# Expert products of a routed attention block: the first product with weights stationary and 512 tokens moving, in tiles of 512 or 384 tokens

## The reference

```python
# attention: 4 batches x 8 heads, 576 positions, 64 wide
scores = q @ k.T / 8;  keep scores >= rowmax - tau;  softmax over the kept;  x = probs @ v
x = x.transpose(0, 2, 1, 3).reshape(2304, 512)
# routed experts: 8 experts, one chosen for each token
logits = x @ w_gate + modality_bias[modality_id];  e_idx = argmax(logits)
for e in range(8):
    mask = e_idx == e
    h = np.maximum(x[mask] @ w1[e], 0.0)          # 512 -> 1024
    out[mask] = gate_w[mask, None] * (h @ w2[e])  # 1024 -> 512
# last stage, all tokens
h = out @ w_in;  g = h * tanh(softplus(h));  return g @ w_out   # 512 -> 2048 -> 512
```

## Time and profile before

| | us |
|---|---|
| median of 3 runs | 943.39 |
| lowest, highest | 942.22, 945.95 |
| the profiled execution, its own time | 944.29 |
| its span | 942.5 |
| PE busy in the span | 911.8 (97%) |
| DVE, ACT, POOL busy | 659.5, 540.9, 474.5 |

### The profile page before, as it was taken

One profiled execution on the slowest core, in us unless ns is written; L12 is line 12 of the kernel. 1 busy time (PEld: TensorE's weight loads), 2 busy tenths in 40 slices (PEclk: granted clock), 3 DMA queues, 4 the chain that ended last, 5 costly groups with the idle time before them and its releaser, 6 DMA issues.

```text
span 942.5 us, 19883 instructions
## 1 busy us (share of the span) xinstructions
PE 911.8 (97%) x7120; PEld 764.8 (81%) x7121; DVE 659.5 (70%) x1179; ACT 540.9 (57%) x1147; POOL 474.5 (50%) x560
## 2 busy tenths in 40 slices
PE   6999999999899999999999989999999999999996
PEld 4777777777678788888877978898889898889985
DVE  7989999998855411111153898888888788788793
ACT  5898898999862322222255465545555455455552
POOL 5232244656512763000000586777776777777884
PEclk9999999999999999999999999999999999999999
DMA  4131337342216563111234100001001000000000
GB/s 131 53 103 53 103 128 260 104 131 69 74 36 200 180 230 81 47 37 46 70 132 177 43 1 3 33 34 34 23 12 35 35 1 1 34 1 1 34 1 34
DMA packets 21940, 66.00 MB, mean 70 GB/s; under 512 B 3553, under 2 KB 3553, under 8 KB 21601
## 3 DMA queue, kind: packets, MB, share of 16 engines
q1 hardware_dynamic: 14512, 39.90, 12.6%
q0 software_dynamic: 4896, 20.00, 6.3%
q10 hardware_dynamic: 2448, 5.01, 1.8%
HBM read 46.63 MB, written 18.27 MB: 69 GB/s over the span
## 4 chain that ended last, share of the span: by engine, by line
PE 61%; DVE 5%; issue 3%; ACT 1%; DMA 1%; ACTq 1%; POOL 0%; DVEq 0%; POOLq 0%; SPq 0%
PE psum L1424 6%; PE psum L1426 6%; PE psum L1425 6%; PE psum L1416 6%; PE psum L1414 6%; PE psum L1415 6%; PE psum L1087 3%; PE psum L1089 3%; PE psum L1088 3%; PE psum L1114 3%; PE psum L1116 3%; PE psum L1115 3%; DVE rr L1536 2%; PE psum L1098 2%; PE psum L1073 1%
## 5 line engine op out<-in xcount | busy, mean ns | idle before, releaser
L1536 DVE RECIPROCAL rr<-rr 128x384 f32<-128x384 f32 x96 | 244.1, 2543 | 10.0 <-ACT rr L1484 10.0
L1362 POOL TENSOR_TENSOR uu<-uu,ex 128x384 f32<-128x384 f32 x96 | 97.5, 1015 | 100.5 <-ACT uu L1478 100.5
L1414 PE MATMUL psum<-x2T_hi,w_in_hi 128*128 128x384 f32 x384 | 131.0, 341 | 4.3 <-DVE gg L1542 2.7
L1416 PE MATMUL psum<-x2T_hi,w_in_lo 128*128 128x384 f32 x384 | 129.7, 338 | 0.0
L1415 PE MATMUL psum<-x2T_lo,w_in_hi 128*128 128x384 f32 x384 | 129.1, 336 | 0.0
L716 DVE TENSOR_SCALAR_CACHE_REDUCE ssb<-psum,tauk 128x576 f32<-128x576 f32 x144 | 112.6, 815 | 21.5 <-PE psum L418 16.5
L564 ACT ACTIVATE prob<-ssb,smin 128x576 f32<-128x576 f32 x144 | 113.0, 787 | 23.6 <-DVE ssb L716 22.8
L1168 DVE TENSOR_TENSOR hT_lo<-psum,hT_hi 128x512 fp32r<-128x512 f32 x38 | 26.3, 691 | 140.5 <-ACT hT_hi L1145 135.5
L1484 ACT ACTIVATE rr<-uu 128x384 f32<-128x384 f32 x96 | 50.5, 526 | 118.8 <-POOL uu L1362 118.8
L1424 PE MATMUL psum<-w_hi,g_hi 128*128 128x512 f32 x288 | 114.5, 398 | 0.1
L1425 PE MATMUL psum<-w_lo,g_hi 128*128 128x512 f32 x288 | 114.0, 396 | 0.0
(11 more groups left out here) (201 smaller groups left out, 2124.0 us busy)
## 6 DMA issues: line engine op xcount, KB each, us to landing
qk<-in_qk_dram SPq DMA_DIRECT2D x15, 640.0 KB, 3.9
vsb<-in_v_dram SPq DMA_DIRECT2D x16, 512.0 KB, 3.7
xrow<-xs ACTq DMA_DIRECT2D x17, 288.0 KB, 2.9
ys<-ysb SPq DMA_DIRECT2D x19, 257.0 KB, 3.2
stage<-in_w_in_dram POOLq DMA_DIRECT2D x16, 256.0 KB, 4.3
wa<-in_wa_dram SPq DMA_DIRECT2D x8, 512.0 KB, 7.8
wb<-in_wb_dram SPq DMA_DIRECT2D x8, 512.0 KB, 11.2
xs<-zrow SPq DMA_DIRECT2D x11, 288.0 KB, 3.1
```

The costliest lines, as they stand in the source:

```text
L1414: pe.matmul(bank_of(n), w_in_hi[:, k, cols], xT_hi[w][:, k], start=(k == 0), stop=False)
L1416: last = pe.matmul(bank_of(n), w_in_lo[:, k, cols], xT_hi[w][:, k], start=False, stop=(k == KT - 1))
L1536: dve.reciprocal(rr[:, n % 4], rr[:, n % 4]).then_inc(r_done, 1)
```

## The change

The first product of the experts is turned around: a block of 128 x 128 of w1 is stationary and up to 512 tokens move, so h comes out with features in rows, as the second product needs it. `turn_h` and its transposes go; the relu and the high half become one ACT operation, `max(h, 0) - high` one DVE operation. Tiles have 512 tokens (`LEAD_W` = 4 blocks of 128) for the lead and 384 (`OTHER_W` = 3) for the others. One tile (instead of three) is worked on early. The rows of a tile are loaded as four blocks, each with its own register load and transfer, always four. There is one buffer for the rows (`xrow`, four blocks), one for the results (`ysb`, four blocks) and a small one for the gates, which are copied over when the previous results have been stored. The halves of the turned x are made by four copies and four subtractions, one for each 128 features, and those of the next tile are made at the end of a tile, after its last first product.

Two loops: one over the lead's tiles, one over the other experts. The w2 pass for the lead goes; POOL now makes the low half of w2. w_in is loaded in four transfers of 1 MB into the place of its low half and split there. The last stage's first chunks of `ys` (`yrow`) now lie where the expert rows lay, so POOL waits for the last turned rows and gates before it loads them, and PE waits for the last expert result before the first product of the last stage, not the eighth. Four blocks of `xs` are cleared instead of three, and the table computation on DVE has some ten small operations more.

```diff
-EARLY = 3
+LEAD_W, OTHER_W = 4, 3
+EARLY = 1
...
-        for i in range(EARLY):
+        for i in range(LEAD_W):
             row = sp.value_load(tab["early"][0:1, i:i + 1], min_val=i * P, max_val=(E - 1) * CAP + i * P)
-            early["load_row"](sp, i, row)
+            early["load_block"](sp, i, row)
...
+    def load_block(eng, j, row):
+        eng.dma_start(xrow[:, j], io["xs"][bass.ds(row, P), :]).then_inc(x_in, 16)
     def load_x(eng, i):
-        load_row(eng, i, eng.value_load(tab["rows"][0:1, 0, bass.ds(i, 1)], min_val=0, max_val=E * CAP - P))
+        eng.wait_ge(x_turned, KT * i)
+        eng.wait_ge(gate_done, i)
+        for j in range(LEAD_W):
+            load_block(eng, j, eng.value_load(tab["rows"][0:1, j, bass.ds(i, 1)], min_val=0, max_val=E * CAP - P))
...
-                pe.matmul(h_bank[:, half, :], xT_hi[:, k], w1h[:, k, c], start=(k == 0), stop=False)
-                pe.matmul(h_bank[:, half, :], xT_hi[:, k], w1l[:, k, c], start=False, stop=False)
-                last = pe.matmul(h_bank[:, half, :], xT_lo[:, k], w1h[:, k, c],
-                                 start=False, stop=(k == KT - 1))
+                pe.matmul(out, w1h[:, k, cols], xT_hi[:, k, q], start=(k == 0), stop=False)
+                pe.matmul(out, w1h[:, k, cols], xT_lo[:, k, q], start=False, stop=False)
+                last = pe.matmul(out, w1l[:, k, cols], xT_hi[:, k, q], start=False, stop=(k == KT - 1))
...
-        def turn_h(i, half):
-            pe.wait_ge(relu_done, 2 * i + 1 + half)
-            for k in range(half_f):
-                f = half * half_f + k
-                last = pe.transpose(ht_bank[:, half, k * P:(k + 1) * P], hid[:, f * P:(f + 1) * P], ident[:])
-            last.then_inc(h_turned, 1)
...
+        def rest_of_tile(i, f0, wide, w1_split, w2_split):
+            for f in range(f0, FT1):
+                if f == FT1 - 1:
+                    turn_x(i + 1, 0)
+                    turn_x(i + 1, 1)
+                up(i, f, wide, w1_split)
+                if f >= 2:
+                    down(i, f - 2, wide, w2_split)
+            turn_x(i + 1, 2)
+            down(i, FT1 - 2, wide, w2_split)
+            turn_x(i + 1, 3)
+            down(i, FT1 - 1, wide, w2_split)
...
+        def tile(i, wide):                    # ACT
+            load_x(act, i + 1)
+            h_hi(i, 0, wide)
+            evacuate_y(i)
+            for f in range(1, FT1):
+                h_hi(i, f, wide)
+            for k in range(KT):
+                x_hi(i + 1, k)
+            move_gates(i)
+            gate_of(i + 1)
...
+        pool.wait_ge(y_stored, 16 * first_rows + 16)
+        pool.wait_ge(x_turned, KT * (tiles + 1))
+        pool.wait_ge(gate_done, tiles + 1)
         for c in range(2):
+            if c == 1:
+                pool.wait_ge(y_stored, 16 * tiles + 16)
+                pool.wait_ge(x_out, KT * (tiles + 1))
...
-            if n == AHEAD - 1:
+            if n == 0:
                 pe.wait_ge(y_out, tiles)
```

More of the change, by code:

```diff
@@ L547, in tensor @@
         rows_out(NS - 2)
[L548 to L555, removed]
+        up(0, 1, LEAD_W, 0, {1: lambda: rows_out(NS - 1)})
+        up(0, 2, LEAD_W, 0)
+        down(0, 0, LEAD_W, 0)
+        ranks(B - 1)
+        up(0, 3, LEAD_W, 0)
+        down(0, 1, LEAD_W, 0)
+        pe.wait_ge(ranks_read, B)
+        rest_of_tile(0, 4, LEAD_W, 0, 0)
     def scalar(act):
@@ L652, in scalar @@
         normalise(NS - 1)
-        h_hi(0, 0)
-        relu(0, 1)
-        x_hi(1)
-        gate_of(1)
[L657 to L668, removed]
+        h_hi(0, 1, LEAD_W)
+        h_hi(0, 2, LEAD_W)
+        gate_exps(B - 1)
+        for f in range(3, FT1):
+            h_hi(0, f, LEAD_W)
+        for k in range(KT):
+            x_hi(1, k)
+        move_gates(0)
+        gate_of(1)
     def vector(dve):
@@ new lines, in gpsimd @@
+        tiles, ranks = counts(pool)
+        first_rows = pool.value_load(tab["counts"][0:1, 2:3], min_val=1, max_val=TILES_MAX)
+        with pool.Fori(1, ranks) as r:
+            for k in range(WP):
+                cols = slice(k * PIECE, (k + 1) * PIECE)
+                pool.wait_ge(w2_hi_done, WP * r + (k + 1))
+                pool.tensor_tensor(w2_lo[:, cols], wb[:, cols], w2_hi[:, cols].bitcast(F32),
+                                   ALU.subtract).then_inc(w2_ready, 1)
+        pool.wait_ge(y_stored, 16 * first_rows + 16)
@@ L1076, in up_half, with turn_x @@
-        def up_half(i, half, split, between={}):
-            c = slice(half * 512, (half + 1) * 512)
-            if half == 0:
-                pe.wait_ge(x_out, i + 1)
-            for k in range(KT):
-                if half == 0:
+        def turn_x(i, k):
+            if k == 0:
+                pe.wait_ge(x_in, 16 * LEAD_W * i + 16 * LEAD_W)
+            if k == KT - 1 or (k == 2 and not first_tile(i)):
+                pe.wait_ge(x_out, KT * i + (1 if first_tile(i) else k - 1))
+            cols = slice(2 * k * HW + E, 2 * k * HW + E + P)
+            for j in range(LEAD_W):
+                last = pe.transpose(x_bank(i, k)[:, j * P:(j + 1) * P], xrow[:, j, cols], ident[:])
+            last.then_inc(x_turned, 1)
@@ L1196, in scalar @@
+        end = lead_end(act)
+        with act.Fori(EARLY, end) as i:
+            tile(i, LEAD_W)
+        w1_high(0, end)
+        with act.Fori(1, ranks) as r:
             first, end = span(act, r)
-            act.wait_ge(t["w2_next"], 16 * WP * (r + 1))
+            act.wait_ge(t["w2_next"], 16 * WP * r)
             for k in range(WP):
@@ L1453, in tensor @@
         pe.wait_ge(w1_ready, WP * (ranks + 1))
-        pe.wait_ge(x_out, tiles + 1)
         for n in range(AHEAD):
@@ L1620, in build @@
+        t["qk"] = over_xT("qk", [P, 2, 2 * S + P])
+        assert over_xT.end <= sb.end
+        over_h, over_h2, x_end = placer(nc, sb.end), placer(nc, sb.end), sb.end
+        t["hT_hi"], t["hT_lo"] = (sb("hT_" + part, [P, H_RING, LEAD_W * P], F32R) for part in ("hi", "lo"))
+        t["ssb"] = over_h("ssb", [P, 2, 2 * S])
         assert over_h.end <= sb.end
-        t["stage"], t["ysb"] = sb("stage", [P, 2, 512]), sb("ysb", [P, YRING, YW])
-        over_work, over_wa, over_wb = placer(nc, work), placer(nc, raw), placer(nc, raw + 4 * WCOLS)
+        t["gates"] = sb("gates", [P, LEAD_W, 2])
```

504 lines of the change are left out of this document (270 added, 234 removed).

## The result

The changed kernel took 952.33 us (median of 4, 950.98 to 952.96) where the kernel before took 944.43 (942.22 to 945.95, 4 runs). The ratio is 1.0084, 95% interval 1.0058 to 1.0109: slower by 0.8%. A second set on another occasion (after_again in the experiments: 953.33 us) gave 1.0090 (1.0062 to 1.0117). The profiled execution has a span of 951.3 us against 942.5: 8.8 us more.

The account below looks back on a forecast made before the run. The prediction took the instructions PE issues as the bound. Its terms, -16.6 + 1.7 - 0.2 - 1.5 + 3.3 + 0.8 + 1.0 + 6.1 + 3.9 + 3.5 = +2.0 us, took 943.4 to 945.4; range 935 to 952.5.

Parts of the forecast that it names:

- The likeliest course: Whole kernel: the summed terms give +2.0 us, 945.4 us, own range 940 to 950.5; chance 0.55.
- rival B: Tile 1's rows take 10 us beside w_in and weights; PE stands 7 us, clock falls again: 953 us; chance 0.18.
- PE's own work: On PE: h transposes go, -16.6 us; four more x transpose groups, +1.7; second expert's first product at 384 columns, -0.2.
- First rows: Before tile 0's x transposes: four loads must land, the fourth issued 3.3 us later, PE's stream behind it: +3.3 us.
- Entering the lead's loop: At tile 1's first h: ACT reads loop bounds and issues four loads before it: +0.8 us.
- Tile 1's rows: Rows loaded behind eight clearing transfers while POOL starts w_in; they land about when PE wants them: +1.0 us.
- Lead to second expert: PE waits 2.9 us for w1 pieces and 3.9 for h behind ACT's loads, less 0.7 now: +6.1 us.
- rival A: Stalls mostly hidden: ACT and SP register loads and transfers overlap, the clock holds; -10.6 us, 933 us; chance 0.22.
- Start of the last stage: Before the last stage's first product: ACT's casts and results delay its x copies, 5.5 us idle against 1.59: +3.9 us.
- Clock: Half clock behind waits at first rows (1.0 us), second expert (1.6) and last stage (0.9): +3.5 us, bounds 0 to 5.

Follow-up runs that it names:

- Experiment 6: Kernel before, with PE's turning of h left out in the loop over tiles (old turned h used): 928.48 us, ratio 0.9853.
- experiment 4: Changed kernel, with the first tile's 512 rows fetched by one register load and one transfer instead of four: 950.40 us, ratio 1.0071.
- Experiments 1 to 3: Changed kernel, holding until tile 1's rows landed: all of w_in, 941.02 us; the second expert's weights, 953.59 us; the last two of four w_in transfers, 945.03 us.
- experiment 8: Also turns_early: changed kernel, w_in after tile 1's rows, one first-row transfer, gates before x casts, last x turn before the last two downs: 933.52 us.
- Experiment 7: Changed kernel, w_in after tile 1's rows, first rows by one transfer, ACT copying gates before x casts in looped tiles: 939.10 us, ratio 0.9956.
- experiment 9: Also fill_wait: changed kernel, with 72 extra identity transposes on PE before its wait for tile 1's rows: 950.11 us, against 953.33 beside it.

## Why the prediction was right, and where it was wrong

The forecast said no change to slightly slower (945.4), with 952.5 as upper end; 952.3 came out. The sign held, and the range held by luck: 0.2 us inside its end, with two of the four runs above it and the second set's median, 953.33, as well. The likeliest course, with its own range of 940 to 950.5, did not come: rival B did, with its place and its mechanism. That its price (953) is so near is luck too: it had the landing, the wait (7 us against 9.25) and the clock too small, and kept the second expert's 6.1, which did not come.

- **PE's own work: right.** -16.6, +1.7 and -0.2, with 46.5 us a tile. Experiment 6 measures the first by itself. The step, not the record's length of 272 ns, was the price.
- **First rows: right in mechanism**, 3.98 for 3.3. Four requests in a row do make them late; they stood 1.24 us apart, not 1.11. But one request for all 512 rows (experiment 4) gave only 1.1 of the 3.98 back, as its own landing was longer. (The 1.9 in the forecast's upper bound stands in no row.)
- **Entering the lead's loop:** 0.66 for 0.8. Right: ACT issued its four loads from 341.51 to 345.29 and the first h followed at 345.40.
- **Tile 1's rows: the step that failed**, +1.0 against 9.25. The forecast put the landing at "about when PE wants them", and argued against B that the rows "are issued first". They were not: POOL's requests began 0.22 us ahead, and all four stood before the third of the rows'. Whether rows requested first would have been spared was not tried. Rival B took 10 us for the landing; 13.4 was measured. The Trainium skill (DMA: Bandwidth & Descriptors, Issuing engines are not separate DMA queues) says that transfers of different issuers share the same engines. Experiments 1 to 3 agree with it: 3.8, 8.5 and 13.4 us with 0, 2.1 and 4.2 MB beside them.
- **Lead to second expert: wrong**, +6.1 against 1.1. The forecast had ACT "begin its four loads with the last cast", after all casts. It issues them while the casts still run (482.09 to 485.45), so the first h follows the last cast at once, at 486.91, and the second stall of 3.9 never came. The first, 2.9 for the pieces of w1, was 1.8. (Where this first wait goes, in experiment 8, a wait for h of 1.70 shows.) This is what rival A said of ACT's loads; its other parts did not hold.
- **Start of the last stage: right in size**, 3.3 for 3.9, but for another reason, if narrowly. The forecast let ACT's casts and results end last; in the trace DMA yrow does, and ACT's path is 0.59 us shorter. Experiment 7 shows that the request, behind the turn and the gates, sets the wait; with it earlier, ACT's path ends last, as forecast.
- **Clock: mis-sized**, 6.3 for 3.5 (1.0 of it a difference). Of the three stalls it was given to, the one at the second expert did not come, and the one at tile 1 was not among them. The first rows' cost was 2.5, not 1.0: the clock was low already when PE restarted, and for 5.0 us more, where the one precedent had 3.2 us of it. That idle time brings it is shown by experiment 9.

So two large errors, a cost of 5.0 us at the second expert that did not come and 8.3 us too little at tile 1, partly cancelled, and the clock's +2.8 came on top. The sum looks better than its terms.

## What to carry to other kernels

When a change makes a load bigger or puts it one tile ahead, list all transfers that are in flight at that moment, whoever issues them, and price the landing by their bytes together; then put the one that nobody needs soon (here w_in, by 200 us) behind the one that PE waits for. A stall on PE costs its length and half of what PE does at the lower clock behind it, here 2.5 and 2.8 us behind waits of 4.25 and 9.25, and 1.7 behind one of 4.43. And look for what a longer unit of work moves back at its ends: the work of the loop gained 16.6 us as worked out, and the three places where rows for the next unit are fetched took 16.5 plus the clock.

## What the runs showed of the hardware that was not expected

- ACT issued the first of four transfers 4.9 us before the casts ahead of it in program order had ended: its register loads and requests did not wait for the engine. But they stood 1.1 us apart, as SP's did, and in the lead's tile, where ACT had no other work, the first h came only behind the fourth (345.40 after 345.29).
- With 4.2 MB requested from 0.22 us ahead on, 1.2 MB of rows took 13.4 us; with nothing beside them 3.8. The first of the four transfers still landed in 3.7. Weights requested behind them cost them nothing (13.2 without them, 13.4 with them).
- The time from PE's restart to the full clock was 5.6 us behind a wait of 9.25, 5.0 behind 4.25 and 3.4 behind 4.43: it does not go by the wait's length alone. Behind waits of 1.64 (turns_early) and 1.38 (fill_wait) it did not fall. With 72 transposes of the identity in the wait of 9.25 the clock stayed at 1.00.
- One transfer of 512 rows took 5.7 us from issue to use, each of four with 128 rows 3.0; the four together, requested 1.24 us apart, were only 1.1 us later.
